# Expert 0 of a routed two-layer network: token rows stationary and 512 weight columns moving, in place of weights stationary and 128 rows moving

## The reference

```python
attn_out = _attn_ref(**attn_kwargs)            # linear attention, 2 x 8 heads, 768 positions
x = attn_out.transpose(0, 2, 1, 3).reshape(1536, 512)
g = x @ moe_w_gate; val = x @ moe_w_val        # gated MLP, 1536 hidden values
x = (g * sigmoid(g) * val) @ moe_w_out
expert_idx = argmax(x @ moe2_w_gate, axis=1)   # one of 8 experts for each token
for e in range(8):                             # 512 -> 1024 -> 512
    h = np.maximum(x[expert_idx == e] @ w1[e], 0.0)
    out[expert_idx == e] = gate_w * (h @ w2[e])
```

## Time and profile before

| | us |
|---|---|
| median of 3 runs | 565.49 (565.02 to 565.71) |
| the profiled execution's own time | 566.59 |
| its span | 564.9 |
| PE busy | 551.9 (98%) |
| PEld busy | 472.5 (84%) |
| DVE busy | 321.1 (57%) |
| ACT busy | 232.2 (41%) |
| POOL busy | 80.0 (14%) |

### The profile page before, as it was taken

How to read it: one execution, slowest core, us unless ns; L and a number is a source line. 1 busy time by engine, 2 the same in 40 slices (tenths; PEclk the granted TensorE clock), 3 DMA queues, 4 the chain that set the end, 5 groups by cost and what they waited for, 6 DMA issues and landing times.

```text
span 564.9 us, 8870 instructions
## 1 busy us (share of the span) xinstructions
PE 551.9 (98%) x3369; PEld 472.5 (84%) x3369; DVE 321.1 (57%) x552; ACT 232.2 (41%) x386; POOL 80.0 (14%) x94
## 2 busy tenths in 40 slices
PE   7999999999999999999999999999999999999994
PEld 7888888888878888887888887899999999999983
DVE  7777445434556545436455665664666665766620
ACT  3115323332453323335335444563465555655410
POOL 5972000000000000000000120012230321312101
PEclk8999999999999999999999999999999999999998
DMA  8886432232223342233143555256564756554001
GB/s 299 299 272 209 175 111 86 83 113 111 68 101 92 114 150 87 81 111 111 56 142 106 219 187 223 77 191 221 161 239 166 275 184 248 200 189 167 13 14 35
DMA packets 18436, 84.50 MB, mean 150 GB/s; under 512 B 3036, under 2 KB 3036, under 8 KB 14816
## 3 DMA queue, kind: packets, MB, share of 16 engines
q1 hardware_dynamic: 13536, 71.35, 36.6%
q0 software_dynamic: 3712, 10.54, 5.3%
q10 hardware_dynamic: 1152, 2.13, 1.0%
HBM read 78.73 MB, written 7.39 MB: 152 GB/s over the span
## 4 chain that ended last, share of the span: by engine, by line
PE 95%; DVE 1%; ACT 1%; issue 0%; DMA 0%; POOL 0%; POOLq 0%
PE bank L643 35%; PE bank L653 17%; PE bank L845 14%; PE bank L855 12%; PE bank L612 2%; PE bank L576 2%; PE bank L585 2%; PE bank L903 2%; PE bank L769 2%; PE bank L883 2%; PE bank L601 1%; PE bank L777 1%; PE bank L834 1%; PE bank L684 1%; PE bank L666 1%; PE bank L896 1%
## 5 line engine op out<-in xcount | busy, mean ns | idle before, releaser
L1158 DVE TENSOR_TENSOR ewl<-stage,ewh 128x1024 fp32r<-128x1024 f32 x64 | 78.0, 1222 | 20.0 <-ACT ewh L947 20.0
L1279 DVE TENSOR_TENSOR sig<-bank,sig 128x512 f32<-128x512 f32 x36 | 24.9, 692 | 99.6 <-ACT sig L992 99.6
L643 PE MATMUL bank<-xh,gvh 128*128 (+1 forms) x288 | 77.1, 390 | 0.0
L643 PE MATMUL bank<-xl,gvh 128*128 (+1 forms) x288 | 77.0, 390 | 0.0
L643 PE MATMUL bank<-xh,gvl 128*128 (+1 forms) x288 | 77.0, 390 | 0.0
L947 ACT ACTIVATE ewh<-stage 128x1024 fp32r<-128x1024 f32 x64 | 67.0, 1052 | 0.2
L992 ACT ACTIVATE sig<-bank 128x512 f32<-128x512 f32 x36 | 21.7, 603 | 105.0 <-PE bank L643 105.0
L643 PEld LDWEIGHTS bank<-xl,gvh 128*128 128x128 f32 x288 | 54.1, 188 | 11.2
L643 PEld LDWEIGHTS bank<-xh,gvh 128*128 128x128 f32 x288 | 54.0, 188 | 11.3 <-issue 0.2
L643 PEld LDWEIGHTS bank<-xh,gvl 128*128 128x128 f32 x288 | 54.1, 188 | 11.2
L653 PE MATMUL bank<-hh,woh 128*128 128x512 f32 x144 | 57.2, 397 | 0.7 <-DVE hl L1158 0.7
(11 more groups left out here) (190 smaller groups left out, 921.7 us busy)
## 6 DMA issues: line engine op xcount, KB each, us to landing
stage<-expert_w SPq DMA_DIRECT2D x28, 1024.0 KB, 4.9
stage<-mlp_w SPq DMA_DIRECT2D x36, 768.0 KB, 4.4
stage<-attn_in SPq DMA_DIRECT2D x24, 512.0 KB, 5.0
stage<-expert_w POOLq DMA_DIRECT2D x8, 512.0 KB, 5.5
x_rows<-x ACTq DMA_DIRECT2D x8, 260.0 KB, 5.1
x_rows<-x SPq DMA_DIRECT2D x4, 260.0 KB, 2.5
out<-ys,idx POOLq DMA_INDIRECT x16, 3.9
gx<-x_rows,idx POOLq DMA_INDIRECT x15, 4.6
```

The source lines that it names most:

```text
L643: last = mm(bank[:, where, :], wt[:, k, :], (xh, xl)[x][:, k, bass.ds(g * GT, GT)], start=(at == 0), stop=(at == 3 * KD - 1))
L1158: V.tensor_tensor(dst, src, high.bitcast(F32), ALU.subtract).then_inc(inc, 1)
L1279: V.tensor_tensor(sig[:, :], bank[:, GATE_BANK, :], sig[:, :], ALU.mult).then_inc(sg_ready, 1)
```

## The change

For both tiles of expert 0 the operands change places. The split rows (`exa`, or `exh` and `exl`) become stationary, and 512 columns of the first weights move through them: four blocks of 128 hidden values at once, which lie 1024 elements apart in `ewh0` and `ewl0`. Each tile has two halves `h` of 12 matmuls. The result stands token by hidden value; ScalarE takes its relu (`relu_half`, into `sig` or `hid`, free by then), TensorE turns it back with four transposes (`turn_half`), and ScalarE and VectorE split that into `turned` (`high_half`, `low_half`). The second products (`half_outward`) are the same 24 matmuls as before.

The order of the other work changes with it. The early tile's transposes move from unit 10 to unit 9 of the last MLP group, and its splitting from unit 11 to unit 10. The first gather of expert 1 waits for the early tile's transposes alone, and not for `expo_ready`. The splits of expert 1's weights are placed anew, three of eight beside the first tile, three more beside the second, two after the split of expert 1's rows.

```diff
@@ gpsimd, first_pass
                 gather_b()
+                pool.wait_ge(gx_read, 1)
+                fetch(gx[0], x2_rows, idx[:, 2:3], gx_landed[0])
+                pool.wait_ge(expo_ready, 1)
+                fetch(gx[1], x2_rows, idx[:, 3:4], gx_landed[1])
                 nc.gpsimd.memset(idx_now[:, :], 0).then_inc(now_ready, 2 * E - 2)
-                gather(1)
@@ tensor
-                    if end and f == NF1 - 2:
+                    if end and f == NF1 - 3:
                         transpose_a()
+            def half_hidden(tile, h, first, last):
+                pe.wait_ge(exl_ready, tile + 1)
+                pe.wait_ge(ewl_ready, NF2)
+                if tile:
+                    pe.wait_ge(ehl_ready, 2 * h + 2)
+                for at in range(first, last):
+                    w, z = split_terms[at // KD]
+                    k = at % KD
+                    rows_now = (exh, exl)[z][0][:, k, P:] if tile else exa[z][:, k, :]
+                    ins = mm(bank[:, H_BANK + h, :].rearrange("p (f i) -> p f i", f=HALF_F), rows_now,
+                             expert_bufs(0)[w][:, h * HALF_F:(h + 1) * HALF_F, k * P:(k + 1) * P],
+                             start=(at == 0), stop=(at == 3 * KD - 1))
+                if last == 3 * KD:
+                    ins.then_inc(eh_psum, 2)
+            def turn_half(tile, h):
+                pe.wait_ge(flat_ready, 2 * tile + h + 1)
+                for f in range(HALF_F):
+                    last = nc.tensor.transpose(bank[:, H_BANK + h, f * P:(f + 1) * P], flat(h)[:, f * P:(f + 1) * P],
+                                               ident[:, :])
+                last.then_inc(turned_psum, 1)
...
-            for f in range(2, NF2 - 3):
-                outward_a(f)
-                hidden_a(f + 2)
-            outward_a(NF2 - 3)
+            half_hidden(0, 1, 8, 12)
+            half_outward(0, 0, 0, 3)
+            turn_half(0, 1)
+            half_outward(0, 0, 3, 12)
+            half_outward(0, 1, 0, 6)
             transpose_b()
-            hidden_a(NF2 - 1)
-            outward_a(NF2 - 2)
-            outward_a(NF2 - 1)
+            half_outward(0, 1, 6, 12)
@@ tensor, first_expert
+                half_hidden(1, 0, 0, 12)
+                half_hidden(1, 1, 0, 4)
+                turn_half(1, 0)
+                half_hidden(1, 1, 4, 12)
+                half_outward(1, 0, 0, 3)
+                turn_half(1, 1)
+                half_outward(1, 0, 3, 12)
+                transpose_rows(1, True)
+                half_outward(1, 1, 0, 12)
@@ scalar
+            def relu_half(tile, h):
+                act.wait_ge(eh_psum, 4 * tile + 2 * h + 2)
+                nc.scalar.activation(flat(h), bank[:, H_BANK + h, :], ACT.Relu).then_inc(flat_ready, 1)
+            def high_half(tile, h):
+                act.wait_ge(turned_psum, 2 * tile + h + 1)
+                copy(turned[0][:, h, :], bank[:, H_BANK + h, :]).then_inc(ehh_ready, 2)
@@ vector
+            def low_half(tile, h):
+                dve.wait_ge(ehh_ready, 4 * tile + 2 * h + 2)
+                V.tensor_tensor(turned[1][:, h, :], bank[:, H_BANK + h, :], turned[0][:, h, :].bitcast(F32),
+                                ALU.subtract).then_inc(ehl_ready, 2)
```

More of the change, by code:

```diff
@@ L155, in bass_linear_attention_mlp_moe @@
         x2 = sb("x2", [P, GTT, ROW], F32, region2)
-        x2f = sb("x2f", [P, KD, GT], F32, region2)
+        region3 = ExitStack()
+        x2f = sb("x2f", [P, KD, GT], F32, region3)
+        region3.close()
+        region3 = ExitStack()
+        turned = [sb(f"turned{z}", [P, 2, GT], F32R, region3) for z in range(2)]
+        region2.enter_context(region3)
         lt = sb("lt", [2 * E, GT], F32, region2)
@@ L242, in bass_linear_attention_mlp_moe @@
         lift_step = sem("lift_step")
-        ea_psum = sem("ea_psum")
-        eah_ready = sem("eah_ready")
-        eal_ready = sem("eal_ready")
+        flat_ready = sem("flat_ready")
+        turned_psum = sem("turned_psum")
         gx_landed = [sem(f"gx_landed{i}") for i in range(2)]
@@ L281, in bass_linear_attention_mlp_moe, with flat @@
         A_BANK, COUNT_BANK = 7, 0
+        HALF_F = NF2 // 2
         split_terms = ((0, 0), (0, 1), (1, 0))
+        def flat(h):
+            return (sig, hid)[h][:, :]
         block = ctx.enter_context(nc.Block())
@@ new lines, in turn_half, with half_outward @@
+            def turn_half(tile, h):
[4 more added lines that the diff above has]
+                last.then_inc(turned_psum, 1)
+            def half_outward(tile, h, first, last):
+                pe.wait_ge(ehl_ready, 4 * tile + 2 * h + 2)
+                for at in range(first, last):
+                    f = at // 3
+                    w, z = split_terms[at % 3]
+                    ins = mm(bank[:, Y_BANK + 1 if tile else A_BANK, 0:DM], turned[z][:, h, f * P:(f + 1) * P],
+                             expert_bufs(0)[w][:, h * HALF_F + f, KD * P:],
+                             start=(h == 0 and at == 0), stop=(h == 1 and at == 3 * HALF_F - 1))
+                if h == 1 and last == 3 * HALF_F:
+                    ins.then_inc(y_psum, 1)
@@ L803, in _ @@
             logit_product(NG - 1)
-            hidden_a(0)
+            half_hidden(0, 0, 0, 4)
             pe.wait_ge(lt_ready, NG)
@@ L812, in _ @@
             rows(NG - 1, GTT - 1, GTT - 1)
-            hidden_a(1)
-            for f in range(2):
-                outward_a(f)
-                hidden_a(f + 2)
+            half_hidden(0, 0, 4, 12)
+            half_hidden(0, 1, 0, 4)
+            turn_half(0, 0)
+            half_hidden(0, 1, 4, 8)
             table()
-            for f in range(2, NF2 - 3):
-                outward_a(f)
-                hidden_a(f + 2)
-            outward_a(NF2 - 3)
+            half_hidden(0, 1, 8, 12)
[3 more added lines that the diff above has]
+            half_outward(0, 1, 0, 6)
             transpose_b()
-            hidden_a(NF2 - 1)
-            outward_a(NF2 - 2)
-            outward_a(NF2 - 1)
+            half_outward(0, 1, 6, 12)
             def transpose_rows(x, first=False):
@@ L1035, in second_half @@
                     unit(g, f, (g, f + 1) if f < NF1 - 1 else None if end else (g + 1, 0),
-                         FIRST_CHUNKS[f - HALF] if end else (), rows_a if end and f == NF1 - 1 else None)
+                         FIRST_CHUNKS[f - HALF] if end else (), rows_a if end and f == NF1 - 2 else None)
             def rows_a():
@@ L1060, in _ @@
             evacuate(NG - 1)
-            relu_a(0)
             for t in range(GTT):
                 rows_out(NG - 1, t, t)
[L1064 to L1067, removed]
+            relu_half(0, 0)
+            high_half(0, 0)
+            split_second_expert(0)
+            relu_half(0, 1)
+            high_half(0, 1)
+            split_second_expert(1)
+            split_second_expert(2)
             rows_b()
-            relu_a(NF2 - 1)
-            split_second_expert(NF2 - 3)
             nc.scalar.activation(expo[:, 0, :], logits_a[:, :], ACT.Exp)
@@ L1074, in first_expert @@
             def first_expert():
[L1075 to L1087, removed]
+                split_second_expert(3)
+                split_second_expert(4)
+                relu_half(1, 0)
+                high_half(1, 0)
+                split_second_expert(5)
+                relu_half(1, 1)
+                high_half(1, 1)
+                act.wait_ge(y_psum, 1)
+                act.wait_ge(gate_ready_x, 1)
+                nc.scalar.activation(ys[0][:, :], bank[:, A_BANK, 0:DM], ACT.Copy,
+                                     scale=gate_now[:, 0, 0:1]).then_inc(y0_ready, 1)
+                tokens(1, 1)
+                split_second_expert(6)
+                split_second_expert(7)
             def tokens(x, par):
@@ L1396, in second_half @@
                          FIRST_CHUNKS[f - HALF] if end else (),
-                         {HALF + 1: slots_a, NF1 - 1: rows_a}.get(f) if end else None)
+                         {HALF + 1: slots_a, NF1 - 2: rows_a}.get(f) if end else None)
             first_half(0)
@@ L1440, in _ @@
             V.tensor_scalar(passes[:, :], mosti[:, :], 8, None, ALU.logical_shift_right).then_inc(slots_ready, 1)
[L1442 to L1447, removed]
+            split_second_expert(0)
+            low_half(0, 1)
+            split_second_expert(1)
+            split_second_expert(2)
+            low(exl[0][:, :, P:], bank[:, ROUTE_BANK, :].rearrange("p (k i) -> p k i", k=KD),
+                exh[0][:, :, P:], exh_ready, 2, exl_ready)
             def tokens(x, par):
@@ L1496, in first_expert @@
             def first_expert():
[L1497 to L1505, removed]
+                split_second_expert(3)
+                split_second_expert(4)
+                low_half(1, 0)
+                split_second_expert(5)
+                low_half(1, 1)
+                tokens(1, 1)
+                split_second_expert(6)
+                split_second_expert(7)
                 dve.wait_ge(y_psum, 2)
```

12 lines of the change are left out of this document (1 added, 11 removed).

## The result

| | before | changed |
|---|---|---|
| median | 565.60 us (565.02 to 565.75, 4 runs) | 556.25 us (555.67 to 556.46, 4 runs) |
| profiled execution, span | 564.9 | 553.9 |
| PE busy | 551.9 | 541.4 |
| PEld busy | 472.5 | 458.9 |

The ratio is 0.9835, 95% interval 0.9818 to 0.9852: 9.35 us faster, where 9.56 were forecast (555.9 predicted, range 554.8 to 559.2). The two spans differ by 11.0, more than the medians. So the comparison is made on the stretch.

A forecast was written before the change was run, and what follows sets the result against it. TensorE was taken to bound the kernel almost throughout. 9.74 + 1.10 - 1.84 + 1.58 (waits that go) - 1.02 (waits that come) = 9.56 us; 565.49 - 9.56 = 555.93 us, range 554.8 to 559.2.

The forecast's parts named there:

- First products: Expert 0's first products: 48 matmuls of 512 columns at 0.227, 10.90 us instead of 20.64, 9.74 less.
- Second products: Expert 0's second products: same 48 matmuls, in longer streams at 0.227 each, 10.90 instead of 12.0 us, 1.10 less.
- Turning back: Sixteen added 128x128 transposes of expert 0's relu result on TensorE, 0.46 us for four: 1.84 us more.
- The wait before the last `out_product`: TensorE's 0.72 us idle before the MLP's last `out_product` goes; 0.76 counted with 0.04 of drift.
- Expert 1's first split: TensorE waits 0.25 us at expert 1's first split of relu, VectorE having weight splits and `ys[1]` ahead of it.
- Course: New order laid out by paces and waits from 352.66 to 389.11, which is 9.56 us before 398.67.
- Gathers: Second tile's gather and expert 1's second fetch land just before TensorE wants them, thin margins costed at nothing.
- rival A: A gather is late and TensorE waits 1.7 us, or 3 if both are: 557.6 to 559; chance 0.12.
- Rival B: Transposes don't overlap, each costs its mean 0.278 us: 2.6 us less gain, 558.5; chance 0.03.
- D: First products' four moving pieces are read at half the column rate: 10.9 us more, 566.8; chance 0.05.
- E: Each first product costs 0.28 us instead of 0.227 because of its moving pieces: 2.5 us, 558.5; chance 0.06.
- C: Clock falls to 1.2 GHz for 5 us in the stretch with more transposes and waits: 2.5 us lost, 558.4; chance 0.03.

The follow-up runs named there:

- four pieces: Changed kernel with each first product of 512 columns issued as four matmuls of 128 columns, same stationary rows loaded for each: 566.32 us.
- operand in one piece: Changed kernel with the first products' moving operand as 512 neighbouring columns (expert 0's values then wrong, same amount of work): 556.19 us.
- version in two pieces: Changed kernel with each first product of 512 columns issued as two matmuls of 256 columns: 556.54 us.
- table sooner: Against a 555.33 us version of the changed kernel with three waits attacked: table behind first four turning transposes, `idx` earlier, second tile's transposes earlier: 556.41 us.

## Why the prediction was right, term by term

- **First products**, 9.74 forecast. The 48 take 11.44 in the chain (0.93 + 2.78 + 0.93 + 1.04 + 3.92 + 1.84), where 10.90 were counted: 9.2 gained. The mechanism was right, and four pieces show that all of it hangs on the width. About 0.28 of the excess is the slow start behind the table (0.11) and behind the wait for the split rows (0.17). The rest is the pace, mis-sized a little, 0.232 for 0.227. It isn't a price of changing between widths. In the timeline the first 512-column matmul behind four transposes takes 0.31 us to the next one's start, but the last transpose took only 0.03 instead of 0.11, and a stream without any change runs no faster. Here are twelve second products, from the first of the two starts to the second, 2.80 / 12 = 0.233:

```profile
367.44 0.63 PE L802 MATMUL bank<-ewh,turned 128*128 128x512 f32 x2
...
370.24 0.60 PE L824 MATMUL bank<-ident,gx 128*128 128x128 f32 x4
```

What makes this pace stays open. The operand's shape, of which no row of before told anything, costs nothing; for that the forecast had a reason but no row.
- **Second products**, 1.10 forecast: 11.15 in the chain (0.70 + 3.48 + 1.39 + 0.70 + 2.09 + 2.79), so 0.85: the same pace of 0.232, against 0.227 counted.
- **Turning back**, 1.84 and two waits of 0.17, together 2.18. Measured 0.44 + 0.64 + 0.44 + 0.64 = 2.16, and 1.77 for sixteen more. The second transposition of each tile stands behind three matmuls that don't need its relu, and not behind the seven that are named under "The change": four of those belong to the sum that the relu waits for.
- **The wait before the last `out_product`**: gone, and worth 0.8 to 1.1 us by itself (0.76, and 0.25 net for the restart and the logits, were counted). Unit 10 bore the copy and split without delay, as worked out: `gate_val` and `out_product` of units 10 and 11 follow each other without a gap.
- **Logits**: 2.01 in the chain, as before the change; 1.82 + 0.23 forecast.
- **Expert 1's first split**: 0.17 (1.54 for 1.37 in the next group of six), 0.25 forecast.
- **Course**: expert 1 was to start 33.42 us after 352.66; it starts after 33.95. The half microsecond lies in the 96 products: 11.44 + 11.15 - 21.80 = 0.79, of which 0.15 had been counted as a wait; the other pieces came out 0.1 shorter together.
- **Gathers**: the second tile's was there 0.35 before TensorE. Expert 1's rows cost no wait in the changed kernel. Their landing isn't in its profile, but from the issue (373.88) to the four transposes that need them (382.20) there are 8.3 us, where 7.9 were forecast. The earlier first fetch, which lets the second be issued 1.3 us sooner, is part of that; the prediction called it no concern. With it gone 6.9 us are left (375.20 to 382.14), and rival A took 0.7 us in a profile. That the 8.3 sufficed is in part luck: one landing in the runs took 8.7.

Rival B was excluded by the changed kernel's chain and by the run with the transposes twice, D and E by the chain's 0.232 us and by the operand in one piece, C by the granted clock. A doesn't occur in the changed kernel's profiles; it does in that of the variant with both fetches late, and in that of the kernel before with the early transposes alone.

## What to carry to other kernels

Read the pace of a matmul stream as time over count: at 128 moving columns it was 0.108 to 0.111, at 256 0.114 to 0.118, at 512 0.227 to 0.232 us, so a product with only 128 rows to move is worth turning round even if its result must be turned back. By the same paces one with 256 rows (experts 1 to 7 here) isn't, which no run tried. When an order is laid out anew, put enough matmuls between a product group and the transposes of its relu to cover the relu and its handovers (0.76 us here: four matmuls, 0.91, covered it, three, 0.68, didn't), and check every gather whose trigger doesn't move as far as its reader does.

## What the runs showed of the hardware that I hadn't expected

The start of the program has two courses, whatever the kernel. The stretches' view of the kernel before, then of the changed one, 10 to 20 us (busy and count by engine, then the granted clock):

```profile
10.00:20.00 10.00, 9.89 (x139) 9.05 (x140) 8.06 (x15) 1.67 (x5) 8.41 (x9) 0.83 0.96 351
```

```profile
10.00:20.00 10.00, 9.50 (x158) 8.47 (x160) 8.61 (x16) 1.98 (x5) 8.39 (x9) 1.00 0.96 379
```

In the first, part of these 10 us ran at 1.2 GHz (mean granted clock 0.83): the same 16 matmuls of 64 columns took 1.12 us there and 0.69 in the changed kernel. Ahead of it TensorE had worked for 6.6 and 6.2 of 10 us, at a clock of 1.00 in both, with waits of 1.8, 0.9 and 0.8 us in the first and 1.8, 1.3 and 0.8 in the second, which doesn't tell the two apart. Unit 10's `out_product` then ends at 352.66 and at 351.64. The change is no cause of it: the version in two pieces and the one with the table sooner, which begin like the changed kernel, have the 0.83 too, and three more profiles have a dip that spreads over the first 20 us (early transposes alone, four pieces, transposes twice). With a dip that `out_product` ends at 351.9 to 352.7 in the profiles, without one at 351.6 to 351.9. That is up to 1 us, as much as most terms of the sum, and the reason to compare stretches and not spans. It isn't all that scatters: executions of the kernel before at a mean clock of 0.997 took from 564.95 to 566.43. What decides on the dip, and what the rest of the scatter is, stays open.

The landing of a gather that is issued while weights are loading took 7.8 us in one kernel and 8.7 in the kernel before with the early transposes alone, beyond the 7.6 that the trace of before had as its longest.
